# Mixture-of-experts tail of a float32 kernel: each tile's down-projection issued one tile later

## The reference, cut to what matters

```
logits = x @ w_gate;  local_gate = sigmoid(x @ w_local)         # 2304 tokens, 512 wide
e[s] = argmax(logits[s]) if s == 0 or local_gate[s] < 0.5 else e[s-1]
h = relu(x[s] @ w1[e])            # 512 -> 1024, 8 experts
out[s] = softmax(logits[s])[e] * (h @ w2[e])                    # 1024 -> 512
```

## Time and profile before

| what | value |
|---|---|
| median of 3 runs | 594.37 us (593.65 to 596.05) |
| the profiled execution: its own time | 596.32 us |
| its span | 594.6 us |
| mean granted TensorE clock | 0.982 of full speed |
| PE busy | 554.7 us (93%) |
| PEld busy | 469.4 us (79%) |
| DVE busy | 310.2 us (52%) |
| ACT busy | 268.5 us (45%) |
| POOL busy | 216.9 us (36%) |
| chain that ended last | PE 90%, DVE 2%, ACT 2%, DMA 2%, issue 2% |

### The profile page before, as it was taken

How to read it: one execution, slowest core, us unless ns; L and a number is a source line. 1 busy time by engine, 2 the same in 40 slices (tenths; PEclk the granted TensorE clock), 3 DMA queues, 4 the chain that set the end, 5 groups by cost and what they waited for, 6 DMA issues and landing times.

```text
span 594.6 us, 12965 instructions
## 1 busy us (share of the span) xinstructions
PE 554.7 (93%) x5189; PEld 469.4 (79%) x5189; DVE 310.2 (52%) x491; ACT 268.5 (45%) x463; POOL 216.9 (36%) x218
## 2 busy tenths in 40 slices
PE   4999999999979999999949999999999999999994
PEld 4888878787868999678838888888888888888883
DVE  3276776767686555285424555621456665542121
ACT  2245556564566621363524556522456555532221
POOL 2019898989979930437410100010000011000100
PEclk9999999999989999999979999999999999999998
DMA  8233635535440000008924665531356666411110
GB/s 308 89 119 119 197 98 180 165 106 187 129 153 2 1 1 2 0 1 247 290 101 139 216 239 167 195 106 53 96 187 192 207 210 208 141 39 49 35 52 21
DMA packets 30231, 75.04 MB, mean 126 GB/s; under 512 B 3311, under 2 KB 3439, under 8 KB 30192
## 3 DMA queue, kind: packets, MB, share of 16 engines
q1 hardware_dynamic: 23536, 58.73, 30.9%
q0 software_dynamic: 3200, 9.46, 4.2%
q10 hardware_dynamic: 3456, 6.32, 3.9%
HBM read 57.94 MB, written 17.61 MB: 127 GB/s over the span
## 4 chain that ended last, share of the span: by engine, by line
PE 90%; DVE 2%; ACT 2%; issue 2%; DMA 2%; POOL 0%; ACTq 0%; SPq 0%; POOLq 0%; DVEq 0%
PE turn L507 10%; PE turn L508 10%; PE turn L509 10%; PE num_ps L507 7%; PE num_ps L508 7%; PE num_ps L509 7%; PE pair_ps L516 6%; PE kv_ps L550 6%; PE num_ps L563 6%; PE pair_ps L697 3%; PE pair_ps L507 3%; PE pair_ps L509 3%; PE pair_ps L508 3%; PE turn L492 2%; PE turn L502 2%
## 5 line engine op out<-in xcount | busy, mean ns | idle before, releaser
L469 POOL DMA_INDIRECT out_rows<-o_sb,meta_cur x22 | 25.5, 1159 | 262.9 <-DVE o_sb L1112 262.9
L443 POOL TENSOR_TENSOR gate<-gate,tap 128x576 f32<-128x576 f32 x64 | 93.1, 1454 | 5.3
L1103 DVE TENSOR_TENSOR h_t<-pair_ps,h_t 128x512 fp32r<-128x512 f32 x44 | 30.4, 692 | 115.3 <-ACT h_t L899 115.3
L967 DVE TENSOR_TENSOR wts<-stage,wts 128x1024 fp32r<-128x1024 f32 x64 | 75.7, 1218 | 10.9 <-ACT wts L842 10.9
L507 PE MATMUL num_ps<-wts,y_t 128*128 128x512 f32 x176 | 72.6, 412 | 1.5 <-DVE y_t L1094 1.5
L507 PE MATMUL turn<-wts,h_t 128*128 128x512 f32 x176 | 73.2, 416 | 0.0
L842 ACT CAST wts<-stage 128x1024 fp32r<-128x1024 f32 x64 | 65.1, 1048 | 12.7 <-PE turn L509 11.1
L508 PE MATMUL num_ps<-wts,y_t 128*128 128x512 f32 x176 | 70.5, 401 | 0.0
L509 PE MATMUL num_ps<-wts,y_t 128*128 128x512 f32 x176 | 70.4, 400 | 0.0
L508 PE MATMUL turn<-wts,h_t 128*128 128x512 f32 x176 | 69.7, 396 | 0.0
L509 PE MATMUL turn<-wts,h_t 128*128 128x512 f32 x176 | 69.6, 395 | 0.0
(11 more groups left out here) (158 smaller groups left out, 1045.7 us busy)
## 6 DMA issues: line engine op xcount, KB each, us to landing
stage<-in_w SPq DMA_DIRECT2D x64, 512.0 KB, 4.6
kq_t<-in_kq SPq DMA_DIRECT2D x16, 576.0 KB, 6.0
sorted_rows<-padrow SPq DMA_DIRECT2D x9, 771.0 KB, 5.8
ysl<-sorted_rows ACTq DMA_DIRECT2D x24, 257.0 KB, 2.7
v_sb<-in_v_aug SPq DMA_DIRECT2D x16, 325.0 KB, 3.1
wout_t<-in_w_out_t SPq DMA_DIRECT2D x1, 1024.0 KB, 8.1
wval_sb<-in_w_val SPq DMA_DIRECT2D x1, 1024.0 KB, 10.1
wout_sb<-in_w_out SPq DMA_DIRECT2D x1, 1024.0 KB, 12.3
```

The lines of the kernel that those rows point to most:

```text
L443: nc.gpsimd.tensor_tensor(g, g, tap[:, t % 2, :], ALU.add).then_inc(conv_step, 1)
L967: nc.vector.tensor_tensor(lo, whole, hi.bitcast(F32), ALU.subtract).then_inc(signal, 1)
```

## The change

In iteration t PE now issues the 24 up matmuls of tile t, then slices 0 to 3 of the down-projection of tile t-1, then all twelve transposes (`turn_y(t+1)`, `turn_h(t,0)`, `turn_h(t,1)`), then slices 4 to 7 of tile t-1. The first iteration has no tile before it; the last down-projection stands behind the nest. ACT and DVE follow: the rounding of `h` moves behind `read_y`, its second half behind `o_ok` of the tile before; DVE's scaling of tile t-1 stands near the end of iteration t; the two columns now go through `meta_next`, `meta_mid` and `meta_cur`, with `meta_got` counting the last move. ACT's weight chunks of a new expert wait for the up-projection of the tile before (`h_ok`) and no longer for its down-projection. No arithmetic is added or removed except for one small copy in each tile.

```diff
             def tile_of(e, t, fresh, _):
-                pe.wait_ge(yt_ok, t + 1)
-                for c in range(CT):
-                    up(0, c)
-                up(1, 0)
-                up(1, 1)
-                turn_h(t, 0)
-                up(1, 2)
-                up(1, 3)
-                turn_y(t + 1)
-                pe.wait_ge(o_read, t + 1)
-                pe.wait_ge(ht_ok, t * 2 + 1)
-                down(0)
-                turn_h(t, 1)
-                down(1)
-                down(2)
-                down(3)
-                pe.wait_ge(ht_ok, t * 2 + 2)
-                for kk in range(4, KT):
-                    ins = down(kk)
-                ins.then_inc(o_ok, 1)
+                up_w = wts[2 * e % UNITS]
+                pe.wait_ge(yt_ok, t + 1)
+                for half in range(2):
+                    for c in range(CT):
+                        if fresh and half == 0:
+                            pe.wait_ge(w_lo, 2 * CPU * e + c + 1)
+                        cols = slice(c * F + half * 512, c * F + (half + 1) * 512)
+                        ins = product(h_ps[half], [y_t[:, i, c, :] for i in range(2)], [up_w[:, i, cols] for i in range(2)],
+                                      c == 0, c == CT - 1)
+                    ins.then_inc(h_ok, 1)
+                owner = e - 1 if fresh else e
+                if owner >= 0:
+                    down(owner, t, range(0, KT // 2))
+                    pe.wait_ge(ht_ok, t * 2 + 1)
+                turn_y(t + 1)
+                for half in range(2):
+                    turn_h(t, half)
+                if owner >= 0:
+                    down(owner, t, range(KT // 2, KT))
+
+            def down(e, done, part):
+                down_w = wts[(2 * e + 1) % UNITS]
+                if part[0] == 0:
+                    pe.wait_ge(o_read, done)
+                    pe.wait_ge(ht_ok, done * 2)
+                else:
+                    pe.wait_ge(ht_ok, done * 2 + 1)
+                for kk in part:
+                    if kk % (KT // CPU) == 0:
                         pe.wait_ge(w_lo, 2 * CPU * e + CPU + kk // (KT // CPU) + 1)
...
             turn_y(0)
-            each_expert(pe, tile_of)
+            total = each_expert(pe, tile_of)
+            down(E - 1, total, range(0, KT // 2))
+            down(E - 1, total, range(KT // 2, KT))
...
             def tile_of(e, t, fresh, chunks):        # scalar
                 if fresh and e >= 1:
-                    act.wait_ge(o_ok, t)
+                    act.wait_ge(h_ok, t * 2)
                 for i in chunks[0:2]:
                     round_weights(i)
                 for half in range(2):
                     act.wait_ge(h_ok, t * 2 + half + 1)
                     nc.scalar.activation(h_sb[:, half * 512:(half + 1) * 512], num_ps[:, half, :], ACT.Relu).then_inc(h_read, 1)
-                    act.wait_ge(th_ok, t * 2 + half + 1)
-                    nc.scalar.copy(h_t[:, 0, half * 4:(half + 1) * 4, :].rearrange("p k x -> p (k x)"),
-                                   proj_ps[half][:]).then_inc(h_hi, 1)
                 for i in chunks[2:3]:
                     round_weights(i)
                 read_y(t + 1)
+                round_h(t, 0)
                 for i in chunks[3:4]:
                     round_weights(i)
+                if not (fresh and e == 0):
+                    act.wait_ge(o_ok, t)
+                round_h(t, 1)
...
             def tile_of(e, t, fresh, chunks):        # vector
                 for i in chunks[0:2]:
                     rest_of_weights(i)
-                for half in range(2):
-                    dve.wait_ge(h_hi, t * 2 + half + 1)
-                    parts = [h_t[:, i, half * 4:(half + 1) * 4, :].rearrange("p k x -> p (k x)") for i in range(2)]
-                    V.tensor_tensor(parts[1], proj_ps[half][:], parts[0].bitcast(F32), ALU.subtract).then_inc(ht_ok, 1)
+                for i in chunks[2:3]:
+                    rest_of_weights(i)
                 dve.wait_ge(yt_copy, t + 1)
-                dve.wait_ge(o_free, t + 1)
-                V.tensor_copy(meta_cur[:], meta_next[:]).then_inc(meta_ok, 1)
+                if fresh and e == 0:
+                    V.tensor_copy(meta_mid[:], meta_next[:]).then_inc(meta_ok, 1)
+                else:
+                    dve.wait_ge(o_free, t)
+                    V.tensor_copy(meta_cur[:], meta_mid[:]).then_inc(meta_got, 1)
+                    dve.wait_ge(meta_got, t)
+                    V.tensor_copy(meta_mid[:], meta_next[:]).then_inc(meta_ok, 1)
                 rest_of_y(t + 1)
-                for i in chunks[2:4]:
+                rest_of_h(t, 0)
+                for i in chunks[3:4]:
                     rest_of_weights(i)
-                dve.wait_ge(meta_ok, t + 1)
-                dve.wait_ge(o_ok, t + 1)
-                V.tensor_scalar(o_sb[:], turn_ps[1][:], meta_cur[:, 1:2], None, ALU.mult).then_inc(o_read, 1)
+                if not (fresh and e == 0):
+                    dve.wait_ge(meta_got, t)
+                    scale_out(t)
+                rest_of_h(t, 1)
...
-            each_expert(dve, tile_of, rest_of_weights)
+            total = each_expert(dve, tile_of, rest_of_weights)
+            dve.wait_ge(o_free, total)
+            V.tensor_copy(meta_cur[:], meta_mid[:]).then_inc(meta_got, 1)
+            dve.wait_ge(meta_got, total)
+            scale_out(total)
```

More of the change, by code:

```diff
@@ L130, in attention_moe_kernel @@
     meta_next = place("meta_next", [P, 2], F32, spot["o_sb"])
-    meta_cur = place("meta_cur", [P, 2], F32, spot["meta_next"])
+    meta_mid = place("meta_mid", [P, 2], F32, spot["meta_next"])
+    meta_cur = place("meta_cur", [P, 2], F32, spot["meta_mid"])
     assert spot["meta_cur"] <= b0
@@ L262, in attention_moe_kernel @@
         meta_ok = sem("meta_ok")
+        meta_got = sem("meta_got")
         out_done = sem("out_done")
@@ L305, in each_expert @@
                 first = last
+            return first
         def weight_chunk(i):
@@ L700, in tile_of @@
             def tile_of(e, t, fresh, _):
[L702 to L711, removed]
@@ L713, in down @@
-                def down(kk):
-                    if fresh and kk % (KT // CPU) == 0:
-                        pe.wait_ge(w_lo, 2 * CPU * e + CPU + kk // (KT // CPU) + 1)
-                    return product(o_ps[:], [h_t[:, i, kk, :] for i in range(2)],
-                                   [down_w[:, i, kk * C:(kk + 1) * C] for i in range(2)], kk == 0, kk == KT - 1)
-                pe.wait_ge(yt_ok, t + 1)
-                for c in range(CT):
-                    up(0, c)
-                up(1, 0)
@@ new lines, in tile_of @@
+                owner = e - 1 if fresh else e
[16 more added lines that the diff above has]
+                    if kk % (KT // CPU) == 0:
+                        pe.wait_ge(w_lo, 2 * CPU * e + CPU + kk // (KT // CPU) + 1)
+                    ins = product(o_ps[:], [h_t[:, i, kk, :] for i in range(2)],
+                                  [down_w[:, i, kk * C:(kk + 1) * C] for i in range(2)], kk == 0, kk == KT - 1)
+                if part[-1] == KT - 1:
+                    ins.then_inc(o_ok, 1)
@@ L903, in tile_of, with round_h @@
                 read_y(t + 1)
+                round_h(t, 0)
                 for i in chunks[3:4]:
                     round_weights(i)
+                if not (fresh and e == 0):
+                    act.wait_ge(o_ok, t)
+                round_h(t, 1)
+            def round_h(t, half):
+                act.wait_ge(th_ok, t * 2 + half + 1)
+                nc.scalar.copy(h_t[:, 0, half * 4:(half + 1) * 4, :].rearrange("p k x -> p (k x)"),
+                               proj_ps[half][:]).then_inc(h_hi, 1)
             each_expert(act, tile_of, round_weights)
@@ L1095, in rest_of_y, with rest_of_h, scale_out @@
                                 y_t[:, 0].rearrange("p c x -> p (c x)").bitcast(F32), ALU.subtract).then_inc(yt_ok, 1)
+            def rest_of_h(t, half):
+                dve.wait_ge(h_hi, t * 2 + half + 1)
+                parts = [h_t[:, i, half * 4:(half + 1) * 4, :].rearrange("p k x -> p (k x)") for i in range(2)]
+                V.tensor_tensor(parts[1], proj_ps[half][:], parts[0].bitcast(F32), ALU.subtract).then_inc(ht_ok, 1)
+            def scale_out(done):
+                dve.wait_ge(o_ok, done)
+                V.tensor_scalar(o_sb[:], turn_ps[1][:], meta_cur[:, 1:2], None, ALU.mult).then_inc(o_read, 1)
             def tile_of(e, t, fresh, chunks):
@@ L1099, in tile_of @@
                     rest_of_weights(i)
-                for half in range(2):
-                    dve.wait_ge(h_hi, t * 2 + half + 1)
-                    parts = [h_t[:, i, half * 4:(half + 1) * 4, :].rearrange("p k x -> p (k x)") for i in range(2)]
-                    V.tensor_tensor(parts[1], proj_ps[half][:], parts[0].bitcast(F32), ALU.subtract).then_inc(ht_ok, 1)
+                for i in chunks[2:3]:
+                    rest_of_weights(i)
                 dve.wait_ge(yt_copy, t + 1)
```

(18 more changed lines are left out.)

## The result

The changed kernel takes 599.75 us (median of 9 runs) against 594.37 us (median of 9 runs). By the medians it is slower by 5.4 us, where 6.3 were forecast (600.7 us). One of its nine runs (798 us) was disturbed; the ratio leaves it out and is 1.0082, with a 95% interval of 1.0057 to 1.0107, which is 4.9 us (3.4 to 6.4) and not quite the quotient of the two medians. The profiled execution took 601.04 us, with a span of 599.3 us against 594.6.

What follows compares the result with a forecast made beforehand. PE's own work was taken to bound the expert stage. The terms -0.4 + 3.4 + 2.2 + 1.1 = +6.3 us, added to the 594.4 us median, gave 600.7 us; range 597.6 to 603.2, for this forecast alone 599.2 to 602.3.

Steps and rivals of the forecast that it cites:

- Nothing to hide: Expert stage: PE waits for nobody after the very first tile, so a latency-hiding order has no wait to remove.
- Merging: Twelve transposes per tile in one group: two groups fewer in 22 tiles, 0.01 us each, 0.4 us gained.
- Rival B: Merged transposes run at the matmul's rate, 0.058 us each; 13 us gained, about 587.5 us; chance 0.07.
- The first tile: Before the second tile, PE stalls for `y_t` behind the third weight chunk and column copies; 3.4 us lost.
- The clock: Behind the first tile's stall, PE's clock falls to half over dense matmuls; 2.2 us lost, bounds nothing to 3.2.
- rival A: The clock holds through the gap before the second tile; 598.5 us; chance 0.22.
- The end: The last down-projection waits for DVE to scale the bank of the tile before; 1.1 us lost.
- Steady waits: Steady tiles: `y_t` comes 2 us early, 1.5 with the slowest scatter; every wait has cover, costed at nothing.
- rival C: Scatter, `meta_got` and chunk rests come over 1.5 us late in tiles with chunks; 7 us, about 607.5 us; chance 0.06.

Runs made afterwards that it cites:

- Run 5: Changed kernel, but from the second tile on its twelve transposes stand in three groups of four again; 598.96 us, ratio 1.0102.
- run 1: Changed kernel, but in the very first tile the third weight chunk's rounding (ACT) and rest (DVE) come behind `y_t` and the first half of `h_t`; 595.85 us.
- run 2: Changed kernel, but in the very first tile only DVE's rest of the third weight chunk stands behind `y_t`; 596.85 us, ratio 1.0038.
- run 6: Kernel before the change, with 28 and 7 extra matmuls while PE waits ahead of the expert stage; 591.47 us, ratio 0.9970.
- run 3: Changed kernel with 12 extra matmuls into an unread bank behind the first tile's transposes, filling the gap; 598.76 us, ratio 1.0080.
- run 8: Changed kernel measured once more without edits, to count executions in which the clock falls; 601.12 us, ratio 1.0105.
- run 4: Changed kernel, but the very last down-projection goes into a PSUM bank of its own, without the wait for DVE's scaling; 599.43 us, ratio 1.0087.
- run 9: Changed kernel, but in every tile with weight chunks the fourth chunk is also rounded and its rest written ahead of `y_t`; 601.28 us, ratio 1.0134.

## Why the prediction was right, and where it was not

- **Nothing to hide.** Right. PE waited nowhere in the steady tiles before, and the new order found nothing to hide there. Steady tiles: 12.507 us against 12.52.
- **Merging: -0.4 us forecast, -0.25 measured in the nineteen steady tiles.** Run 5 shows it in isolation. The matmul rows alone, with their 0.31 us step behind each group, would have misled; the row of the weight loads settled it. The price of 81 ns that the Trainium skill states for a load and matmul pair of 128 columns (page "TensorE: Matmul & The Clock Gate", section "Back-to-back issue gap") is not seen: twelve transposes still take 1.30 us, 0.108 each. Rival B falls.
- **The first tile: 3.4 us forecast, 3.2 measured** (gap 3.11). The chain was the one written down, and runs 1 and 2 took it apart.
- **The clock: 2.2 us forecast, on the path in the likeliest case.** The mechanism is right: idle time of PE brings the clock down (runs 6 and 3), and with the gap filled none of seven executions lies in the upper group (run 3). The size where it occurs is 2.7 us, since thirteen matmuls of the second tile and not twelve ran at half speed, and the first of them took 0.59 us to the next. What failed is the either-or between forecast and rival A: a gap of this length brings the clock down in some executions and not in others. The upper group of the sixteen executions (run 8) has a mean of 601.6 us, the lower one 598.2. The forecasts of the two cases were 600.7 and 598.5, and the median lies between.
- **The end: 1.1 us forecast, 1.3 measured** (run 4). The term was short by 0.25 us: PE followed 0.25 us after the scaling and not 0.06 (585.39 to 585.64), and its next step was slow too. The 0.06 was read where PE waited for a value that stands in the code; behind the loops it computes it into a register first (L731). That this makes the difference is a reading of the order, not tested.
- **Steady waits (rival C).** Not there: the cover was 1.86 us or more in every steady tile (2 forecast, 1.5 at worst), and in run 9 another 1.2 us of work was put ahead of `y_t` without an effect.

The sum was 6.3; the profiled execution lost 6.98 in the stage, the median 5.4. That the total came out close is in part luck: the clock's term was too small where it occurs, and it occurs in part of the executions only. The two errors offset each other, and a median of eight or nine executions can fall on either side of 600 us (599.75 here, 601.12 in run 8).

## What to carry to other kernels

Before a pipeline is made deeper, look whether the bound engine waits at all in its steady state; here it did not, so the change had some tenths of a microsecond to gain there (0.25 measured) and could only lose at its ends, where each stage lacks a partner. An order of work is designed for the steady tile, but the first one has the same side work and none of the cover: the weight chunk that costs nothing in thirteen tiles cost 2.5 us in one. And price an idle gap of TensorE twice, once for itself and once for the clock behind it: here filling some 8 idle microseconds ahead of the stage (6.9 and 1.5) was worth 2.3 us, the only real gain found (591.5 us).

## What was not expected of the hardware

The same gap, 3.11 us to the hundredth, ended at half clock in the changed kernel's two profiles and at full clock in run 5's. A gap near the end of the attention stage shows it too, in code that the change does not touch: 2.67 us in the kernel before, with a mean clock of 0.52 over the 7 us from 173.50, and 2.66 us in the changed kernel, whose same stretch had 0.76. How far the clock's fall and rise lie from the gap, and how long it stays at half, differs between executions of the same code. So the loss behind a gap is a spread of times, and a median over few runs moves with it by one or two microseconds.

```profile
171.50:173.50 2.00, 0.02 (x2) 1.00 0.00 0
173.50:180.50 7.00, 6.67 (x101) 0.76 0.00 0
```

These are two stretches of the changed kernel, with PE alone: length, busy time and count, granted clock, DMA share, GB/s. Cut where the clock changes, the time at half behind this gap is 3.4 us in the changed kernel, where the fall comes 1.2 us after the gap's end at 173.48 (first line below), and 6.9 us in the kernel before, where it comes 0.5 us ahead of the end at 174.32 (second line):

```profile
174.70:178.10 3.40, 3.40 (x47) 0.50 0.00 0
...
173.80:180.70 6.90, 6.38 (x79) 0.51 0.00 0
```

What sets the start of the expert stage in a single execution (306.5 to 308.8 us with the same code) was not followed up; falls like these are one part of it at most.
